# Thirty-three idle products between the others, and the seventh product's weights back on the common address phase, in a kernel of pooled attention and two feed-forward layers

## The reference

```
B, H, S, D = 8, 8, 576, 64
k_p, v_p = k, v averaged over groups of 8 positions        # 72 keys
attn = softmax(q @ k_p.T / sqrt(D));  x = attn @ v_p       # x: (4608, 512)
h = x @ w_in;  g = maximum(0.01 * h, h);  x = g @ w_out            # 512 -> 2048 -> 512
h = x @ w2_in; g = h * clip(h + 3, 0, 6) / 6; out = g @ w2_out     # 512 -> 2048 -> 512
```

## The kernel before

| | streaming columns | weights |
|---|---|---|
| layer 1, L1796 | xs 1 | ring 2 |
| layer 1, L1742 | g 1 | wout 2 |
| layer 2, L1796 | xs 2 | ring 3 |
| layer 2, L1742 and L1883 | wout, w_sums 2 | g, gs 3 |
| layer 1, r = 6 | xs 1 | ring 1 |
| layer 2, r = 6 | xs 2 | ring 2 |

## Time and profile before

### The profile page before, as it was taken

How to read it: one execution, slowest core, us unless ns; L and a number is a source line. 1 busy time by engine, 2 the same in 40 slices (tenths; PEclk the granted TensorE clock), 3 DMA queues, 4 the chain that set the end, 5 groups by cost and what they waited for, 6 DMA issues and landing times.

```text
span 1677.0 us, 40112 instructions
## 1 busy us (share of the span) xinstructions
PE 1665.6 (99%) x13914; PEld 1644.5 (98%) x13914; DVE 1122.1 (67%) x2159; ACT 676.4 (40%) x1427; POOL 429.5 (26%) x451
## 2 busy tenths in 40 slices
PE   9999999999999999999999999999999999999998
PEld 8999999999999999999999999999999999999998
DVE  6668777686776767664555666676767676667665
ACT  5454443233333333332223444444344434343443
POOL 4346552021211112112526471111111111111100
PEclk9999999999999999999999999999999999999999
DMA  7747878678686777858679998898989898989894
GB/s 225 252 144 224 277 248 267 222 229 265 203 270 203 237 250 210 272 171 291 225 258 359 315 325 314 286 331 284 331 283 326 283 330 280 327 283 333 286 309 156
DMA packets 228572, 447.94 MB, mean 267 GB/s; under 512 B 23872, under 2 KB 48448, under 8 KB 219200
## 3 DMA queue, kind: packets, MB, share of 16 engines
q1 hardware_dynamic: 228416, 445.74, 79.9%
HBM read 379.58 MB, written 66.06 MB: 266 GB/s over the span
## 4 chain that ended last, share of the span: by engine, by line
PE 96%; DVE 2%; issue 1%; ACT 1%; DMA 0%; POOL 0%; SPq 0%; DVEq 0%; ACTq 0%
PE ps_h L1796 40%; PE ps_y L1742 36%; PE ps_y L1883 5%; PE ps_att L1883 4%; PE ps_att L1920 2%; PE ps_h L1742 2%; PE ps_att L1902 2%; PE ps_att L1733 1%; PE ps_att L1734 1%; PE ps_att L1735 1%; DVE prob L1561 0%; DMA k_raw<-in_kT 0%; DVE gate L1396 0%; DVE row_max L1542 0%; PE ps_y L1934 0%
## 5 line engine op out<-in xcount | busy, mean ns | idle before, releaser
L1796 PE MATMUL ps_h<-xs_hi,ring 128*128 128x256 f32 x3808 | 812.0, 283 | 2.3 <-DVE h L1462 1.6
L1796 PEld LDWEIGHTS ps_h<-xs_hi,ring 128*128 128x128 f32 x3808 | 644.3, 190 | 6.8 <-issue 4.9
L1796 PE MATMUL ps_h<-xs_lo,ring 128*128 128x256 f32 x1904 | 534.0, 280 | 0.0
L1796 PEld LDWEIGHTS ps_h<-xs_lo,ring 128*128 128x128 f32 x1904 | 358.8, 188 | 0.0
L1142 ACT ACTIVATE g_hi<-gate 128x512 fp32r<-128x512 f32 x288 | 182.0, 632 | 384.3 <-DVE gate L1396 202.9
L1742 PE MATMUL ps_y<-g_hi,wout_hi 128*128 128x256 f32 x1152 | 322.5, 280 | 0.6 <-DVE y_stage L1458 0.6
L1742 PE MATMUL ps_y<-g_hi,wout_lo 128*128 128x256 f32 x1152 | 321.9, 279 | 0.0
L1742 PE MATMUL ps_y<-g_lo,wout_hi 128*128 128x256 f32 x1152 | 321.8, 279 | 0.0
L1742 PEld LDWEIGHTS ps_y<-g_hi,wout_hi 128*128 128x128 f32 x1152 | 219.3, 190 | 0.9 <-DVE y_stage L1458 0.8
L1742 PEld LDWEIGHTS ps_y<-g_lo,wout_hi 128*128 128x128 f32 x1152 | 216.8, 188 | 0.0
L1742 PEld LDWEIGHTS ps_y<-g_hi,wout_lo 128*128 128x128 f32 x1152 | 216.6, 188 | 0.0
(11 more groups left out here) (153 smaller groups left out, 2858.2 us busy)
## 6 DMA issues: line engine op xcount, KB each, us to landing
ring<-w_in_split SPq DMA_DIRECT2D x920, 256.0 KB, 3.9
w_sums<-w_out_sums SPq DMA_DIRECT2D x64, 1024.0 KB, 6.1
w_in_split<-ring SPq DMA_DIRECT2D x56, 256.0 KB, 3.7
w_in_split<-stage SPq DMA_DIRECT2D x56, 256.0 KB, 3.8
k_raw<-in_kT SPq DMA_DIRECT2D x32, 288.0 KB, 3.9
q_raw<-in_qT SPq DMA_DIRECT2D x32, 288.0 KB, 5.7
v_raw<-in_v SPq DMA_DIRECT2D x32, 288.0 KB
x0T<-x_stage SPq DMA_DIRECT2D x32, 288.0 KB, 4.2
```

The costliest lines, as they stand in the source:

```text
L1796: mm = pe.matmul(banks[BANK_OF[r]], a, b[:, r, c, :], start=r in OPENS and c == 0 and n == 0, stop=c == 1 and n == 2, skip_group_check=True)
```

## The change

It has two parts. `LAST_AT` is gone, so that the slot of r = 6 has the phase of the other six. And `descend(layer)` puts three products on PE, once in each of the tiles 7 to 17: after the parts r = 0 to 2 of step 0 and the output products behind them, in T = 9 in step 2. They read 256 columns and 128 weights from `wout` at varied offsets and add to 256 columns of `ps_att` that nothing reads any more (in tiles 7 to 9 no product uses this bank, from T = 10 on its other half is used). No semaphore is waited for or raised.

```diff
-LAST_AT = 48
...
-            r = q % PRODUCTS
-            at = r * 4 * P + STREAM_AT * second + (LAST_AT if r == PRODUCTS - 1 else 0)
+            at = q % PRODUCTS * 4 * P + STREAM_AT * second
...
+            def descend(layer):
...
+                row = wout[0][0][:, 0]
+                for k in (1, 2, 3):
+                    columns = 16 * ((layer - 2 - k) % 4)
+                    weights = HN + 16 * ((layer - 1 - k) % 4)
+                    pe.matmul(ps_att[:, 1, HN:N], row[:, weights:weights + P],
+                              row[:, columns:columns + HN], start=False, stop=True,
+                              skip_group_check=True)
...
                 part(T, i, 2, attention)
                 lagging(2, 0, 3)
                 place(1)
+                if T >= ATT_TILES and i == (2 if T == TILES else 0):
+                    descend(layer)
                 part(T, i, 3, attention)
...
                     pair_part(*back(2), S1)
                     pair_part(*back(2), S4)
+                if i == 0:
+                    descend(2)
                 part(T, i, 3, attention)
```

## The result

The changed kernel takes 1651.37 us (median of 4 runs, 1650.04 to 1652.64) where the one before takes 1679.29 in the same comparison; the ratio is 0.9834, 95% interval 0.9816 to 0.9851. The profiled execution took 1650.04 us, its span 1648.2. The forecast was 1649 us, between 1641 and 1667, and faster with a chance of 0.91.

A forecast was written before the change was run, and what follows sets the result against it. PE's products times their distance were taken to bound the kernel, with PE busy 99% of the span. The sum was 1678.8 - 34 + 4.2 + 0.8 + 4.3 + 1.5 - 6.5 = 1649.1 us, range 1641 to 1667.

The forecast's parts named there:

- distance over 113.3 ns, T = 7 to 17, stalls aside: In tiles 7 to 17, 7,452 products go from wide (117.9 ns apart) to close (113.3 ns), saving 34 us.
- of it left: tile 9: In the first two steps of tile 9, some 190 products stay wide until the call in step 2: 0.8 us.
- of it left: stalls behind a call that end wide: At step 2, six of eight tiles stall, two in seven end wide, 2.5 us each: 4.3 us lost.
- of it left: stalls at tile starts that end wide: At tile starts in T = 7 to 17: no such term in the forecast's sum, listed as 0.
- the 33 products with their changes: Calls in tiles 7 to 17: the added products and four phase changes per call cost 4.2 us together.
- stalls growing, T = 7 to 17: At step 2 of eight tiles, PE arrives earlier and waits longer: 0 to 6.4 us, taken as 1.5 us.
- tiles 0 to 6: In tiles 1 to 6, close stretches no longer end at r = 6: 7.5 us less 1 us, 6.5 us saved.
- its two steps: In tiles 7 to 17: calls end close, and without r = 6's own phase only stalls end close stretches; 34 us.
- The rival that a call ends wide because it is like r = 6: At calls in tiles 7 to 17: calls end wide or throw close to wide; 1668.5 us, chance 0.16.
- rows 2 to 5: Profile rows of PE's product distances before the change, said to differ by 4.6 ns where phases alone differ.

The follow-up runs named there:

- e3_flat: Against the changed kernel: the three products of each call read at the phases of their neighbours, with no step down; 1668.73 us.

## Why the prediction was right

Against the terms of the sum, with distances taken product by product from the starts of the trace. This is the profiled execution, 1650.04 us, the fastest of the four; the median lies 1.3 us higher.

| term | forecast, us | measured, us |
|---|---|---|
| distance over 113.3 ns, T = 7 to 17, stalls aside | 34 | 34.5 before, 5.7 after |
| of it left: tile 9 | 0.8 | 0.8 |
| of it left: stalls behind a call that end wide | 4.3 | 3.9 (T = 13 at step 2, T = 17 at step 5) |
| of it left: stalls at tile starts that end wide | 0 | 0.6 (5 x 28 products) |
| the 33 products with their changes | 4.2 | 4.1 |
| stalls growing, T = 7 to 17 | 1.5 | 0.7 |
| tiles 0 to 6 | 6.5 | 4.9 |

The measured column gives 34.5 - 5.7 - 4.1 - 0.7 + 4.9 = 28.9 us, against 28.8 of the spans. Of the 5.7 us that are left, 0.4 stand in no row.

**The mechanism held in its two steps.** r = 6 with its own phase ended close stretches: with it, the calls are worth nothing (1681.1), without it close stretches run on, 688 products in tile 8 (and 880 across the start of tile 8 with flat calls). And a call ends close. The one case that the earlier trace rows showed, a single change from wide, was a fair guide to a call of four changes in a row. The case that it did not show, a call that comes in close, came out as assumed, 16 of 16, and that was luck: three products at one down, from close, ended wide in three of three.

**The reason that I gave for it did not hold.** The prediction said that the four changes "end on the phases on which they began, so no upward change undoes them". One product down and straight up again does as well, so does one product up, and so do the weights alone. A return up does end wide behind six products, as the earlier trace rows has it, and for a close stream behind three. So direction is not what decides. What does, in terms of the two streams of reads, stays open; the runs give the table above and no mechanism beneath it. The rival that a call ends wide because it is like r = 6, with the weights one phase down against the columns ahead of them, is refuted by the calls themselves: three down has this relation four times in a call and ended close 41 times of 41.

**A reading that was wrong.** The prediction said that rows 2 to 5 differ at phases that alone differ. The long wide stretches of the earlier trace rows and the close one of the earlier trace rows have the same phases from product to product; they differ in what had gone before. That is what makes this a state, and why a change of phases in a few products can pay over hundreds.

**Stalls.** The right total came of errors that cancel in part. I had two wide endings in seven from before, where all seven stalls met a wide stream; the share for a close stream is 68 of 132. Against that there were three stalls at step 2, not six. And stalls at the start of a tile are new: none in before, in seven of the tiles 10 to 17 of the changed kernel, 0.13 to 0.25 us each. Five end wide, and the call 28 products later mends it, which makes the place of the call in step 0 worth more than I saw.

**A wait that I had not named.** In T = 7 PE stalls twice, 1.04 us together, for a sum of ACT's that frees its bank. A timeline of all engines there:

```profile
780.55 0.42 ACT L1083 ACTIVATE stage<-s_sum 128x256 fp32r<-128x256 f32 x1 [2.55 <-DMA w_in_split<-stage]
780.56 0.28 PE L1750 MATMUL ps_y<-g_hi,wout_lo 128*128 128x256 f32 x1
780.87 0.36 ACT L1295 ACTIVATE p<-ps_h 128x256 f32<-128x256 f32 x1
...
781.38 0.36 PE L1804 MATMUL ps_h<-xs_hi,ring 128*128 128x256 f32 x1 [0.55 <-ACT p L1295]
```

ACT's queue is in order: the copy that PE needs stands behind a split of the second layer's weights, which waits 2.55 us for a stage buffer's store to land. The chain ahead of that stall has these pieces (start, us, what):

```profile
772.06 2.81 POOL stage L934 x4
774.87 5.57 DMA w_in_split<-stage
```

Most of it is POOL and DMA work, 8.4 us of it, which closer products of PE do not shorten. It may also be why more calls gained nothing in tiles 7 and 8; this was not tried apart.

**Tiles 0 to 6** gave 4.9 us, 0.9 of it ahead of tile 1, where I had counted nothing. Tiles 1 to 6 gave 4.0 of the 6.5 forecast: the close state does live on behind r = 6 of steps 0 and 6, but the attention's stages also turn the stream wide, and there are now wide stretches behind them, mostly of 24 and of 56 or 57 products, where before most or all of these products had been close. I had allowed 1 us of 7.5 for these; 3.5 are missing.

## What to carry to other kernels

When PE is busy 99% of the time, divide stretches by their products before believing it is at its best: two distances at one clock, here 113.3 and 117.9 ns, mean a state that can be set. In this kernel it paid to keep the places of both operands modulo 256 bytes the same from product to product, and to put one short pattern of other places in each tile, where stalls recur; ten more such calls gained nothing that could be measured. Test such a pattern from both states, since some only turn the state over. Once PE's products stand 4% closer, look at in-order queues of other engines whose chains end in a transfer.

## What the runs showed of the hardware

- Matmuls of 128 weights by 256 columns of the short format run in one of two lasting distances at the same granted clock of 1.00, 113.3 or 117.8 to 117.9 ns. The wide one lasted for 1,324 products, the close one for 880 (e3_flat, across the start of tile 8).
- The Trainium skill, "SBUF — State Buffer", section "Who interferes with whom", has PE's two read ports independent and PE waiting on no one. By that, where operands start should not matter. The flat calls and the walking calls are the same products on the same buffers, at ratios of 0.9943 and 0.9834, and differ in nothing but offsets of 64 to 192 bytes, so here the measurement decides: the starts do matter. Whether it is the two ports that disturb each other, no run shows.
- The weights one phase lower, with the columns in place, cost 120 ns a product while they last.
- With a short pattern of phases the outcome was the same in all calls of its kind, 150 in all, given the state ahead of it, and the same three reads in the opposite order had another outcome (three down, three up). A stall that found PE close left it wide 68 times of 132.
